# First groups of a fused convolution and gated MLP taken in another order, with the first loads reordered

## What is computed

```
w   = softmax(weight_gen, over the 7 taps)
a   = sum over k of w[token, head, k] * x[token - 6 + k, head's 24 channels]    (zeros ahead of a sequence)
h   = a @ w_in                     # [16384, 192] x [192, 2048]
g   = h if h >= 1, 0 if h <= -1, else (h + 1)^2 / 4
out = g @ w_out                    # [16384, 2048] x [2048, 192]
```

## Time and profile before

| | |
|---|---|
| median of 3 runs | 1261.16 us (1260.84 to 1261.38) |
| span of the profiled execution | 1259.3 us |
| PE busy | 1209.8 us (96%) |
| ACT busy | 898.3 us (71%) |
| DVE busy | 818.9 us (65%) |
| POOL busy | 697.0 us (55%) |
| DMA | 51.59 MB, mean 41 GB/s |

### The profile page before, as it was taken

How to read it: one execution, slowest core, us unless ns; L and a number is a source line. 1 busy time by engine, 2 the same in 40 slices (tenths; PEclk the granted TensorE clock), 3 DMA queues, 4 the chain that set the end, 5 groups by cost and what they waited for, 6 DMA issues and landing times.

```text
span 1259.3 us, 21159 instructions
## 1 busy us (share of the span) xinstructions
PE 1209.8 (96%) x6932; PEld 1094.7 (87%) x6932; DVE 818.9 (65%) x1434; ACT 898.3 (71%) x1773; POOL 697.0 (55%) x450
## 2 busy tenths in 40 slices
PE   0699999999999999999999999999999999999998
PEld 0578999999999999999999999999999999999987
DVE  1886666666666666666666666666666666666565
ACT  0567777777777777777777777777777777777776
POOL 2496555775555775555776555676555676555500
PEclk9999999999999999999999999999999999999999
DMA  3311111001111101111101111101111100110000
GB/s 116 105 36 48 49 48 48 27 20 47 47 47 47 44 3 47 47 47 47 47 0 47 47 47 47 47 8 39 47 47 47 47 20 27 47 47 12 13 13 13
DMA packets 17426, 51.59 MB, mean 41 GB/s; under 512 B 1800, under 2 KB 8068, under 8 KB 17408
## 3 DMA queue, kind: packets, MB, share of 16 engines
q1 hardware_dynamic: 17264, 51.25, 11.9%
q10 hardware_dynamic: 144, 0.11, 0.0%
HBM read 38.77 MB, written 12.58 MB: 41 GB/s over the span
## 4 chain that ended last, share of the span: by engine, by line
PE 93%; SPq 3%; DVE 3%; DMA 1%; ACT 1%; issue 0%; DVEq 0%
PE slot L581 46%; PE acc L601 44%; PE slot L566 2%; SPq L240 1%; SPq L255 1%; DMA out_raw<-in_moe_w_out 1%; SPq L252 1%; DVE slot L472 1%; DVE gate_low L478 1%; DVE out_parts L515 0%; DVE in_main_low L508 0%; SPq L258 0%; DVE in_rest_low L508 0%; ACT gate_high L375 0%; SPq L223 0%
## 5 line engine op out<-in xcount | busy, mean ns | idle before, releaser
L601 PE MATMUL acc<-out_parts,gate_high 128*128 128x384 f32 x2048 | 616.4, 357 | 6.0 <-DVE gate_low L478 5.9
L478 DVE TENSOR_TENSOR gate_low<-slot,gate_high 128x512 fp32r<-128x512 f32 x512 | 353.7, 691 | 398.9 <-ACT gate_high L375 398.6
L601 PE MATMUL acc<-out_parts,gate_low 128*128 128x192 f32 x2048 | 513.7, 251 | 0.5 <-DVE gate_low L478 0.5
L364 ACT ACTIVATE half_relu<-slot 128x512 f32<-128x512 f32 x512 | 307.7, 601 | 288.5 <-PE slot L581 288.4
L601 PEld LDWEIGHTS acc<-out_parts,gate_high 128*128 128x128 f32 x2048 | 384.9, 188 | 27.1 <-DVE gate_low L478 8.4
L601 PEld LDWEIGHTS acc<-out_parts,gate_low 128*128 128x128 f32 x2048 | 390.3, 191 | 17.9 <-DVE gate_low L478 0.7
L472 DVE SCALAR_TENSOR_TENSOR slot<-slot,square 128x512 f32<-128x512 f32 x512 | 353.0, 690 | 3.9 <-ACT square L370 3.9
L370 ACT ACTIVATE square<-half_relu 128x512 f32<-128x512 f32 x512 | 325.2, 635 | 0.0
L375 ACT ACTIVATE gate_high<-slot 128x512 fp32r<-128x512 f32 x512 | 304.0, 594 | 25.6 <-DVE slot L472 25.4
L301 POOL TENSOR_TENSOR conv<-x_in,tap_w 128x768 f32<-128x768 f32 x31 | 47.8, 1542 | 482.3 <-DVE tap_w L462 468.4
L301 POOL TENSOR_TENSOR tap<-x_in,tap_w 128x768 f32<-128x768 f32 x186 | 289.6, 1564 | 0.0
(11 more groups left out here) (41 smaller groups left out, 493.4 us busy)
## 6 DMA issues: line engine op xcount, KB each, us to landing
x_in<-in_x SPq DMA_DIRECT2D x30, 960.0 KB
out<-out_sb SPq DMA_DIRECT2D x32, 384.0 KB, 2.6
gen_in<-in_weight_gen SPq DMA_DIRECT2D x31, 112.0 KB, 2.3
out_raw<-in_moe_w_out SPq DMA_DIRECT2D x4, 384.0 KB, 9.9
in_main<-in_moe_w_in SPq DMA_DIRECT2D x4, 256.0 KB, 4.7
in_rest<-in_moe_w_in SPq DMA_DIRECT2D x8, 128.0 KB, 7.6
x_in<-in_x SPq DMA_DIRECT2D x1, 768.0 KB
x_in<-in_x SPq DMA_DIRECT2D x4, 139.5 KB
```

What stands on the lines that cost most here:

```text
L364: nc.scalar.activation(half_relu[n % 2][:], tile_slot(pair, b, n)[:], ACT.Relu, scale=0.5, bias=0.5).then_inc(relu_done, 1)
L478: nc.vector.tensor_tensor(gate_low[n % 4][:], tile_slot(pair, b, n)[:], gate_high[n % 4][:].bitcast(F32), ALU.subtract).then_inc(gate_low_ ...
L601: ins = nc.tensor.matmul(dst, stationary, moving, start=(n == 0 and j == 0), stop=(n == NT - 1 and j == 1))
```

## The change

The first two pairs change places in time: pair 0 now handles run tokens 8 to 15 and pair 1 tokens 0 to 7 (`at_pair`), in loads and stores alike. So the first loads of x are plain ones, and the edge rows belong to pair 1 (`is_edge`): their loads are issued with that pair's reloads, the 31 partitions of a sequence in two transfers of 15 and 16, and GpSimd zeroes the four partitions ahead of each convolution of pair 1 (`pad_x`). The initial loads are x of group 0, w_in chunks 0 and 1, w_out chunk 0, gate weights of group 1, w_in chunks 2 and 3, x of group 1, w_out chunks 1 to 3. ScalarE's rounded copies of w_out chunks 1 to 3 move: chunk 1 behind the exponential of group 1, chunks 2 and 3 behind tiles 2 and 4 of group 0. The first tile of each group waits for the parts of the turned input one by one, ahead of the products that read them. SyncE's loop begins at pair 3 with pairs 0 to 2 written out.

```diff
+OUT_HIGHS_AFTER = {2: 2, 4: 3}
...
+        def at_pair(pair):
+            if isinstance(pair, int) and pair < 2:
+                return 1 - pair
+            return pair
+        def is_edge(pair):
+            return isinstance(pair, int) and pair == 1
+        EDGE_X = 1 + 2 * B
...
                 for s in range(B):
                     lo = s * SEQ_PARTS
-                    sp.dma_start(flat[lo + 1:lo + SEQ_PARTS, 0:before * D],
-                                 x_runs[lo:lo + SEQ_PARTS - 1, (RUN - before) * D:RUN * D]
-                                 ).then_inc(x_loaded[b], 16)
+                    for a, z in ((1, half), (half, SEQ_PARTS)):
+                        sp.dma_start(flat[lo + a:lo + z, 0:before * D],
+                                     x_runs[lo + a - 1:lo + z - 1, (RUN - before) * D:RUN * D]
+                                     ).then_inc(x_loaded[b], 16)
...
+            load_x(0, 0)
+            load_in(0)
+            load_in(1)
+            load_out(0)
+            load_gen(0, 1)
+            load_in(2)
+            load_in(3)
+            load_x(0, 1)
+            load_out(1)
+            load_out(2)
+            load_out(3)
             def reload(pair, b):
                 wait_conv(sp, pair, b, 2)
                 load_gen(pair, b)
-                load_x(pair, b)
+                if is_edge(pair):
+                    load_edge_x(b)
+                else:
+                    load_x(pair, b)
...
-            wait(eng, x_loaded[b], pair, 16, 16 * FIRST_X)
-            if is_first(pair):
-                eng.wait_ge(x_padded, 2 * B)
+            wait(eng, x_loaded[b], pair, 16, 16 if is_first(pair) else 16 * EDGE_X)
+            if is_edge(pair):
+                eng.wait_ge(x_padded, B * (b + 1))
...
+            def pad_x(b):
+                wait_conv(pool, 0, b)
+                for s in range(B):
+                    lo, done = s * SEQ_PARTS, b * B + s
+                    if done:
+                        pool.wait_ge(x_padded, done)
+                    nc.gpsimd.memset(x_in[b][lo:lo + 1, 0:PAD - b * TOK, :], 0.0).then_inc(x_padded, 1)
...
                     for b in range(2):
+                        if is_first(pair):
+                            pad_x(b)
                         convolve(pool, nc.gpsimd, pair + 1, b)
...
             out_high(0)
-            out_high(1)
             turned_top(0, 0, 0)
             turned_top(0, 0, 1)
             exponent(0, 1)
-            out_high(2)
-            out_high(3)
+            out_high(1)
...
                         squared(pair, b, n)
+                        if b == 0 and is_first(pair) and n in OUT_HIGHS_AFTER:
+                            out_high(OUT_HIGHS_AFTER[n])
...
                 if n == 0:
-                    wait(pe, turned_low_done, pair, 4, 2 * b + 2)
+                    wait(pe, turned_high_done, pair, 4, 2 * b + 1)
...
                 for j, (w, xt) in enumerate(products):
+                    if n == 0 and j == 2:
+                        wait(pe, turned_low_done, pair, 4, 2 * b + 1)
+                    if n == 0 and j == 3:
+                        wait(pe, turned_low_done, pair, 4, 2 * b + 2)
```

More of the change, by code:

```diff
@@ L214, in slot_free @@
                 wait(eng, turned_low_done, pair, 4, 2 * (b + 1) + k + 1)
-        FIRST_X = 1 + B
+        def at_pair(pair):
[5 more added lines that the diff above has]
+        EDGE_X = 1 + 2 * B
         block = ctx.enter_context(nc.Block())
@@ L221, in load_gen @@
             def load_gen(pair, b):
-                at = (pair * 2 + b) * (TOK * HK)
+                at = (at_pair(pair) * 2 + b) * (TOK * HK)
                 sp.dma_start(gen_in[b][:].rearrange("p t k -> p (t k)"),
@@ L226, in load_x, with load_edge_x @@
             def load_x(pair, b):
-                at = ((pair * 2 + b) * TOK - PAD) * D
+                at = ((at_pair(pair) * 2 + b) * TOK - PAD) * D
                 sp.dma_start(x_in[b][:].rearrange("p t d -> p (t d)"),
                              x_runs[:, bass.ds(at, (TOK + PAD) * D)]).then_inc(x_loaded[b], 16)
-            def load_first_x(b):
+            def load_edge_x(b):
                 before = PAD - b * TOK
+                half = SEQ_PARTS // 2
                 flat = x_in[b][:].rearrange("p t d -> p (t d)")
@@ L239, in load_first_x, with load_in @@
                     lo = s * SEQ_PARTS
-                    sp.dma_start(flat[lo + 1:lo + SEQ_PARTS, 0:before * D],
-                                 x_runs[lo:lo + SEQ_PARTS - 1, (RUN - before) * D:RUN * D]
-                                 ).then_inc(x_loaded[b], 16)
+                    for a, z in ((1, half), (half, SEQ_PARTS)):
+                        sp.dma_start(flat[lo + a:lo + z, 0:before * D],
+                                     x_runs[lo + a - 1:lo + z - 1, (RUN - before) * D:RUN * D]
+                                     ).then_inc(x_loaded[b], 16)
             def store(pair, b):
                 wait(sp, out_summed, pair, 2 * TOK, TOK * (b + 1))
-                at = (pair * 2 + b) * (TOK * D)
+                at = (at_pair(pair) * 2 + b) * (TOK * D)
                 sp.dma_start(out_runs[:, bass.ds(at, TOK * D)],
                              out_sb[b][:].rearrange("p t d -> p (t d)")).then_inc(out_free[b], 16)
-            load_first_x(0)
-            for c in range(W_CHUNKS):
+            def load_in(c):
                 sp.dma_start(in_main[:, c * CW:(c + 1) * CW], w_in[0:P, c * CW:(c + 1) * CW]
@@ L256, in _, with load_out @@
                                  w_in[P:D, c * CW:(c + 1) * CW]).then_inc(in_loaded[c], 16)
-            for c in range(W_CHUNKS):
+            def load_out(c):
                 sp.dma_start(out_raw[:, c * CT:(c + 1) * CT, :], w_out_tiles[:, c * CT:(c + 1) * CT, :]
                              ).then_inc(out_w_loaded[c], 16)
[L260 to L263, removed]
+            load_x(0, 0)
[9 more added lines that the diff above has]
+            load_out(3)
             def reload(pair, b):
@@ L276, in body @@
                         reload(pair + 1, b)
-            over_pairs(sp, body)
+            for pair in range(3):
+                body(pair)
+            with sp.Fori(3, PAIRS - 1) as pair:
+                body(pair)
+            body(PAIRS - 1)
             store(PAIRS - 1, 0)
@@ L328, in _ @@
         def _(pool):
[L330 to L336, removed]
             nc.gpsimd.memset(ident[:], 0.0).then_inc(ident_done, 1)
@@ L391, in take_cross @@
                                          ).then_inc(cross_copied, 1)
-            act.dma_start(gen_in[0][:].rearrange("p t k -> p (t k)"), w_runs[:, 0:TOK * HK]
-                          ).then_inc(gen_loaded[0], 16)
+            act.dma_start(gen_in[0][:].rearrange("p t k -> p (t k)"),
+                          w_runs[:, 2 * TOK * HK:3 * TOK * HK]).then_inc(gen_loaded[0], 16)
             exponent(0, 0)
```

## The result

The kernel after takes 1238.03 us (1237.82 to 1238.25, 4 runs) against 1261.0 before in the same call: ratio 0.9818, 95% interval 0.9804 to 0.9832. It is 23.0 us faster; forecast were 23.7 (1237.4). The profiled span fell from 1259.3 to 1236.5 us.

A forecast was written before the change was run, and what follows sets the result against it. TensorE bounds the steady part, out of reach; the start waits for x through one DMA engine. 22.1 + 3.4 - 0.8 - 1.0 = 23.7 us gained gives 1237.4 us, range 1235.0 to 1241.0.

The forecast's parts named there:

- The bound and the first x load: Start of kernel: one plain x load replaces edge transfers on one DMA engine; first convolution ends 22.1 us sooner.
- C: End of the first convolution, the mark later times are counted from: 42.0 us before, forecast 19.9.
- +0.7: Start: delay of the first softmax step because more x bytes share the engines with the gate weights; 0 to 1.6 us.
- The softmax steps: Start, ahead of the first convolution: the chain from first softmax step to ready taps takes 3.0 us.
- The weights at nothing: Start: weight loads cost 0, covered by softmax and first convolution, with 3 us to spare at the slower rate.
- The sign I gave: Start, sign that weights aren't late: ScalarE's conversions of input chunk 3 end before 18 us.
- From C to the first gate: First group: gate at C+6.3 instead of C+9.75, two out conversions no longer ahead of relu; gain 3.4 us.
- the conversions in group 0: Conversions moved behind tiles 2 and 4: VectorE waits for the later gate copy, one charged, -0.8 us (0 to -1.7).
- GpSimd becomes late: Turn of group 2: memsets between GpSimd's first two convolutions make TensorE wait 1.0 us (0 to 2.4).
- the rows of contended products: GpSimd's memsets: stretched 16% like products beside VectorE, 4.2 us would become 4.9 and TensorE's wait 1.7.
- The rest at nothing: Pair 1's edge loads, their split and the added first-tile waits: 0, at most 0.02 us a group.
- part 1: First x load: one 960 KB load over 128 partitions replaces five transfers, four on one engine; 22.1 us gained.

The follow-up runs named there:

- e1: Kernel before with only the split: 31 rows of each edge transfer go as 15 and 16, nothing reordered; 1236.84 us.
- e2: Kernel after with the exchange of the first pairs alone: edge transfers of 31 rows, loads, conversions and first-tile wait in the old order; 1238.60 us.
- e4: Kernel after with the first gate weights issued by SyncE ahead of x, in place of ScalarE beside x; 1235.89 us.
- e5: Kernel after with ScalarE's output weight conversions in their old places; 1238.35 us.
- e7: Kernel after with the edge groups as the third pair instead of the second, so the memsets fall into a pause of GpSimd; 1237.47 us.
- e3: Kernel after with edge transfers of 31 rows in pair 1, one transfer a sequence; 1238.39 us.
- e6: Kernel after with one wait ahead of each group's first tile, as before the change; 1237.94 us (1237.13 to 1240.38).
- e9: Kernel of e1 (groups in old order) with first gate weights issued by SyncE ahead of x, conversions and first-tile waits as after; 1236.60 us.
- e8: e7 with first gate weights issued ahead of x and the four input chunks loaded ahead of the output chunks; 1234.35 us.

## Why the prediction was right, step by step

**The bound and the first x load.** One engine carrying 558 KB was the stall. Shown twice, by e1 and e2. The size of the step was off: C moved by 21.0 us, not 22.1. The mis-sized term is "+0.7" for the gate weights. They landed 1.9 us later than before, not 0.7. e4 shows that it was contention. I had counted only x beside them, 1.6 us at most; SyncE's input chunks, issued from 1.21 us on, shared the engines too. The softmax steps took 2.75 us from there, where I had 3.0.

**The weights at nothing.** Right, with 1.6 us to spare ahead of the first turned copy. The sign I gave, the last input chunk converted before 18 us, was wrong by 1.4 us: conversion ended at 19.40. e4 shows how thin the cover was.

**From C to the first gate.** 4.2 us in place of 3.4. The copies began at C+0.74, not C+1.22, because the eight transposes ahead of them took 1.09 us, and 1.75 before; why, no row shows (the clock is 1.00 in both). The rest is that ScalarE's instructions start about 0.1 us before the one ahead of them ends, and I had added them end to end. Nor do the moved conversions make most of the 4.2: with them in their old places (e5) the gate stands at C+6.33, already 3.4 us sooner against C than before, since ScalarE no longer waits for an out chunk behind C (2.6 us before). For the conversions in group 0 I charged 0.8; from first gate to last turn it grew by 1.1 (34.77 against 33.63). The size is near, the mechanism was not mine: VectorE's wait for the gate copy of tile 2 grew by 0.3 only (0.93 from 0.66), and its first weight difference behind the first gate took 1.51 us in place of 0.79, beside GpSimd. Together the last turn of group 0 came 3.0 us earlier against C where I had 2.6.

**GpSimd becomes late.** Right in mechanism and near in size. The memsets took 4.41 us with their waits, near the 4.4 I had, and not stretched to 5.1 as the rows of contended products would have it. Two of VectorE's weight differences stand beside them:

```profile
53.82 0.67 DVE L540 TENSOR_TENSOR in_rest_low<-in_rest,in_rest_high 128x512 fp32r<-128x512 f32 x1
...
55.77 0.95 DVE L547 TENSOR_TENSOR out_parts<-out_raw,out_parts 128x768 fp32r<-128x768 f32 x1
```

The Trainium skill (SBUF — State Buffer, Who interferes with whom) has it that a GpSimd instruction that only writes doesn't meet VectorE's two-input work. The trace agrees: neither difference is longer than with GpSimd idle (0.69 at 21.48 and 0.95 at 24.13), and the memsets keep 1.05 to 1.07 us each. The first convolution began at C+5.6, not C+6.1, and grew by 0.75 us, not 0.4; the second shrank by 1.64, not 0.9; and the turn could have come 0.4 us earlier against C than I had it. TensorE waited 0.8 us where I had 1.0, so these errors nearly cancel, which is luck. e7 gave the 0.8 back.

**The rest at nothing.** e3 confirms it for the transfers in pair 1. The added waits in every group cost nothing that can be seen, though e6's scatter leaves some tenths open.

So 21.0 + 4.2 - 1.1 - 0.8 = 23.3, by the ends of the turn 23.1; the errors in C and in the first gate, 1.1 less and 0.8 more, nearly cancel. The stall, its size and the late GpSimd were foreseen; that the sum came within 0.7 us is in part luck.

**What I didn't see** is that part 1's own mechanism had a cheaper cure. I wrote that the split is worth nothing in time, which holds for its new place. In the old place it alone gains 24.2 us. The rest of the change, as made, costs 1.3 us on top of it. About 1.0 of this stands at the turn of group 2, which starts at 78.00 in e1 and at 78.97 after, although the last turn of group 0 starts at the same time in both (61.26 and 61.32): TensorE waits for a GpSimd whose memsets moved from an idle stretch to a busy one. For the other 0.3 no row shows a place. With the memsets in a pause and the gate weights first, the exchange gains 2.2.

## What to carry to other kernels

When a stretch shows a DMA share of one engine, look at the number of rows of its transfers before reordering anything: the same edge rows in four transfers of 31 rows cost 24 us more here than in eight of 15 and 16 (e1), and these still 2.0 us more than one plain load (e9 against e8). When work moves from an idle stretch of an engine to a busy one, look at who waits at the end of that engine's next chain; and give the smallest load that everything hangs on a place ahead of the large ones, since it shares the engines with whatever is issued beside it (3.4 us in e4).

## What was not expected of the hardware

- Gate weights of 112 KB issued beside x landed 5.5 us after their issue, and 2.1 us after it when issued 0.45 us ahead of x on the same queue (e4).
- TensorE's clock fell to its lower level after 1.73 us of idleness in the profiled run of e6 (mean 0.83 over 20 to 30 us), and in e1 and e2 after 1.7 us it did not there.
- A VectorE instruction of 0.95 us took 2.18 when a GpSimd product had started 0.18 us ahead of it, and the product took 2.33 in place of 1.54 when it started second. A first gate 0.5 us earlier (26.55 against 27.05 in e5) brought the last turn of group 0 no sooner (61.32 against 61.18).
- Not only differences with two inputs are stretched: the softmax step `gen_sum_eps`, 0.18 us with GpSimd idle, took 1.72 us between GpSimd's products in group 0, in the kernel before (at 68.58) as after (at 43.81).
